# Attention ahead of two expert layers: constant products on TensorE in three of its waits

## The chip, the cores and the metric

One NeuronCore of a Trainium2 chip runs one program from start to end. The metric is the device time of that program in microseconds (us); lower is better. Every time below is from one core, and the rows of the trace are from one profiled execution.

## The reference, cut to what matters

The program computes three things in a row: a gated linear attention (written as a recurrence over 768 steps), and two layers of 8 experts each. Only the first one is touched.

```python
B, H, S, D = q.shape                       # 4, 8, 768, 40
for t in range(S):
    m_new = np.maximum(f_gate[:, :, t] + m, i_gate[:, :, t])
    f_stab = np.exp(f_gate[:, :, t] + m - m_new)
    i_stab = np.exp(i_gate[:, :, t] - m_new)
    m = m_new
    C = f_stab[:, :, None, None] * C + i_stab[:, :, None, None] * np.einsum('bhd,bhe->bhde', vt, kt)
    n = f_stab[:, :, None] * n + i_stab[:, :, None] * kt
    h_tilde = np.einsum('bhde,bhe->bhd', C, qt)
    denom = np.maximum(np.abs(np.einsum('bhd,bhd->bh', n, qt)[:, :, None]), 1.0)
    y[:, :, t] = 1.0 / (1.0 + np.exp(-o_gate[:, :, t])) * h_tilde / denom
...
x = y.transpose(0, 2, 1, 3).reshape(B * S, H * D)      # 3072 tokens x 320
x = moe(x)      # logits = x @ w_gate; tokens to 8 experts of equal size, in order of the logits
return moe2(x)  # logits; each token to its best expert, times its softmax weight
```

## The kernel before, in words

**Stages.** The program is a row of blocks, one after the other, with a barrier between them: a small block that makes the constants (an identity `ident` and a tile of ones `ones_b`, 128x128, bf16), the attention, the first expert layer, the second one. This case is about the attention and about the border to the first expert layer.

**The attention, cut into units.** The 768 steps are worked in 6 chunks of 128 tokens (NC = 6). In each chunk there are 8 units (UPC = 8), one for every four of the 32 batch-head pairs, which makes 48 units. For a unit TensorE does, by its functions' names: `decay_rows` (4 products into `p_G`), `scores` (4 wide products of queries and keys into `p_S`), `outputs` (8 products of scores and values, 4 with the state `C`, 8 for the new state, into `p_O`); after every even unit `x_transposes` (3 transposes of the finished rows `xs` into `p_L`) and after every odd one `logits` (6 small products: the logits of the first expert layer). A matrix product in f32 takes more than one instruction's worth of passes; the trace shows it as a longer one or as two.

**The order.** `step(c, k)` issues, on TensorE: `decay_rows(k + 2)`, `scores(k + 1)`, `outputs(k)`, then the transposes or the logits. `steps` runs two lead-in steps, a loop over the first five chunks, and the last chunk written out. TensorE works strictly in the order in which its instructions are issued. VectorE turns `p_G` into log weights (line 368), ScalarE takes their exponentials (300, 303), GpSimd weights the values and decays the state, VectorE multiplies the scores with the weights (377), and after `outputs` reads the result out (391 to 405), and GpSimd scales it and gates it into `xs` (268, 273). SP loads each next chunk's tiles and stores the finished rows.

**The start.** Ahead of the units the gates are worked into `col`, `G` and `G_parts` by VectorE and GpSimd. TensorE waits for `G` and `col`, transposes both in 12 small transposes (lines 435, 436), and then waits for the rest: the constants, the bf16 parts of `G` (`parts_done`), the copy `colT` (`colT_done`), the exponentials `eG` (`eG_done`, ScalarE, line 328) and the gate weights. Only then do `decay_rows(0)` and the rest follow.

**The end.** After the last unit's `outputs` and `logits` TensorE waits until VectorE and GpSimd have finished the last rows (`y_done`), transposes them (line 495), waits until ScalarE has copied the transposes out (`xT_done`, lines 309 and 310), and multiplies the last logits (line 502). VectorE copies these (line 412), the block ends, and the first expert layer starts with VectorE's `best` (884) and TensorE's pivots (1242), then the counting products (1248).

**Constant products that are there already.** The first expert layer has a function `busy(n)` of its own (line 1239) that multiplies the tile of ones by itself, 512 columns wide, into a bank that nobody reads; it is used inside its search rounds, ahead of its experts and at its end. The second layer has six such products at its start (line 1736).

Of the kernel before, what the change touches and what calls it, by code (L numbers as in the profile page):

```python
# [14 lines left out]
P = 128  # L15
# [5 lines left out]
HU = 4  # L21
# [25 lines left out]
def unit(c, k):  # L47

    return c + k // UPC, k % UPC, c * UPC + k


def wait_done(eng, sem, n):

    eng.wait_ge(sem, n + 1 + LEAD)


def steps(eng, step):

    step(0, -2, False)
    step(0, -1, False)  # L60
    with eng.Fori(0, NC - 1) as c:
        for k in range(UPC):
            step(c, k, False)
    for k in range(UPC):
        step(NC - 1, k, True)
# [42 lines left out]
def attention(nc, a, sh):  # L108

    with ExitStack() as ctx:  # L110
# [27 lines left out]
        p_G, p_S, p_O, p_L = bank[1:3], bank[3:5], bank[5:7], bank[7]  # L138
# [64 lines left out]
        def _(pool):  # L203
# [52 lines left out]
            def decayed_state(c, k):  # L256
                _, k, u = unit(c, k)
                wait_done(pool, eGl_done, u)
                wait_done(pool, C_done, u - QB)
                nc.gpsimd.tensor_tensor(Cd[:, k % QB, :, :], C[:, k, :, :].rearrange("p r (j e) -> p (r j) e", e=V1),  # L260
                                        eGl[:, k % QB, :].unsqueeze(2).to_broadcast([P, HU, V1]), ALU.mult).then_inc(Cd_done, 1)
# [30 lines left out]
        def _(act):  # L292
# [3 lines left out]
            def weights(c, k):  # L296
                _, k, u = unit(c, k)
                wait_done(act, C_done, u - QB)
                wait_done(act, D_done, u)
                nc.scalar.activation(eGl[:, k % QB, :], p_G[k % 2][:, :].rearrange("p (h t) -> p h t", t=P)[:, :, P - 1],  # L300
                                     ACT.Exp).then_inc(eGl_done, 1)
                w = W[:, k % QB, :, :].rearrange("p h t -> p (h t)")
                nc.scalar.activation(w, w, ACT.Exp).then_inc(W_done, 1)
# [29 lines left out]
        def _(dve):  # L333
# [29 lines left out]
            def log_weights(c, k):  # L363
                _, k, u = unit(c, k)
                w = W[:, k % QB, :, :].rearrange("p h t -> p (h t)")
                wait_done(dve, mask_done, u)
                wait_done(dve, G_psum, u)
                nc.vector.tensor_tensor(w, p_G[k % 2][:, :], w, ALU.add).then_inc(D_done, 1)  # L368
# [59 lines left out]
        @block.tensor  # L428
        def _(pe):
            for x in pe_sems:  # L430
                pe.sem_inc(x, LEAD - (x is xT_psum or x is L_psum))
            pe.wait_ge(G_done, 1)
            pe.wait_ge(col_done, 1)
            for c in range(NC):
                nc.tensor.transpose(p_L[:, c * BH:(c + 1) * BH], col[0:BH, c * P:(c + 1) * P], ident[0:BH, 0:BH])
                mm = nc.tensor.transpose(p_L[:, (NC + c) * BH:(NC + c + 1) * BH], G[0:BH, c * P:(c + 1) * P], ident[0:BH, 0:BH])
            mm.then_inc(gates_T, 1)
            pe.wait_ge(consts, 4)
            pe.wait_ge(zeroed, 2)
            pe.wait_ge(parts_done, 3)  # L440
            pe.wait_ge(dg, 3)
            pe.wait_ge(colT_done, 1)
            pe.wait_ge(eG_done, 1)
            pe.wait_ge(in_wg, 16)

            def decay_rows(c, k):

                c, k, u = unit(c, k)
                wait_done(pe, D_done, u - 2)
                wait_done(pe, eGl_done, u - 2)  # L450
                pe.sem_inc(pe_carry, 1)
                for h in range(HU):
                    bh = k * HU + h
                    mm = nc.tensor.matmul(p_G[k % 2][:, h * P:(h + 1) * P], pick_row[:, bh:bh + 1].to_broadcast([3 * BH, P]),
                                          G_parts[:, bass.ts(c, P)], start=True, stop=True)
                mm.then_inc(G_psum, 1)

            def scores(c, k):
                c, k, u = unit(c, k)
                b, par = k // 2, k % 2  # L460
                pe.wait_ge(in_qk[b], c * (16 * QLOADS) + 16 * QLOADS)
                pe.sem_inc(pe_carry, 1)
                wait_done(pe, P_done, u - 2)
                for r in range(PR):
                    pair = k % 2 * PR + r
                    mm = nc.tensor.matmul(p_S[par][:, 2 * r * P:(2 * r + 2) * P], kT[:, b, pair, :],  # L466
                                          qD[:, b, pair, :, :].rearrange("p j t -> p (j t)"), start=True, stop=True)
                mm.then_inc(S_psum, 1)

            def outputs(c, k):  # L470
                u = c * UPC + k
                b, h0, par = k // 2, k % 2 * HU, k % 2
                op = p_O[par]
                wait_done(pe, P_done, u)
                pe.wait_ge(in_v[b], c * 16 + 16)
                wait_done(pe, num_done, u - 2)
                wait_done(pe, C_done, u - 2)
                wait_done(pe, wv_done, u)
                for h in range(HU):
                    nc.tensor.matmul(op[:, h * V1:(h + 1) * V1], Pm[:, par, h, :], v[:, b, h0 + h, :], start=True, stop=True)  # L480
                for r in range(PR):
                    mm = nc.tensor.matmul(op[:, (HU + 2 * r) * V1:(HU + 2 * r + 2) * V1], qT[:, b, k % 2 * PR + r, :], C[:, k, r, :],
                                          start=True, stop=True)
                for h in range(HU):
                    mm = nc.tensor.matmul(op[halves[h % 2], (2 * HU + h // 2) * V1:(2 * HU + h // 2 + 1) * V1],
                                          k_[:, b, (h0 + h) * D:(h0 + h + 1) * D], wv[:, k % QB, h, :], start=True, stop=True)
                mm.then_inc(O_psum, 1)

            def x_transposes(c, k):

                i, b = c * B + k // 2 - 1, (k // 2 - 1) % B
                wait_done(pe, y_done, c * UPC + k - 1)
                wait_done(pe, L_done, i - 1)
                for j, (k0, kn) in enumerate(KT):
                    mm = nc.tensor.transpose(p_L[0:kn, j * P:(j + 1) * P], xs[:, b, k0:k0 + kn], ident[:, :])
                mm.then_inc(xT_psum, 1)

            def logits(c, k):
                i = c * B + k // 2 - 1
                pe.wait_ge(xT_done, 2 * i + 2 + 2 + LEAD - 1)  # L500
                for j, (k0, kn) in enumerate(KT):
                    mm = nc.tensor.matmul(p_L[:, 3 * P:3 * P + NE], xT[0:kn, j, :], wg[0:kn, 0, j, :],
                                          start=j == 0, stop=j == len(KT) - 1)
                mm.then_inc(L_psum, 1)

            def step(c, k, last):
                if not (last and k + 2 >= UPC):
                    decay_rows(c, k + 2)
                if not (last and k + 1 >= UPC) and k + 1 >= 0:
                    scores(c, k + 1)  # L510
                if k >= 0:
                    outputs(c, k)
                    if k % 2 == 0:
                        x_transposes(c, k)
                    else:
                        logits(c, k - 1)

            steps(pe, step)
            x_transposes(NC - 1, UPC)
            logits(NC - 1, UPC)  # L520


# [1389 lines left out]
```

## Time and profile before

| | us |
|---|---|
| three runs | 804.33, 804.60, 815.23 |
| median of the three | 804.6 |
| the profiled execution, its own time | 811.87 |
| its span in the trace | 810.2 |
| TensorE busy, share of the span | 707.8 (87%) |
| VectorE busy | 549.8 (68%) |
| attention, in the span | to about 208.4 |

The span is what the trace covers; 1.7 us of the execution's own time lie outside it. The profiled execution took 7.3 us more than the median of the runs. A busy TensorE says that an instruction was in flight, not that the array worked at its full speed: the same instruction can take twice as long at the lower of its two clock levels (1.2 and 2.4 GHz).

### The profile page before, as it was taken

The page shows a single profiled execution, that of the slowest core. Times are in us where ns is not written, and L with a number is a line of the kernel's source. Part 1 is how long each engine was busy: PE and PEld are TensorE (multiplying, and loading weights), DVE is VectorE, ACT ScalarE, POOL GpSimd, SP SyncE. Part 2 cuts the span into 40 slices and gives each one's busy share as a digit, 9 for nine tenths or more (in the row PEclk, how much of TensorE's full clock was granted, in tenths as well). Part 3 has the DMA queues.
Part 4 walks back from the last instruction along what each step waited for, and adds up shares of the span by engine and source line. Part 5 has one row for each costly group of instructions (what it writes and reads, how often), then busy time and mean ns, then how long its engine had stood idle before and what let it go on. Part 6 is the DMA issues. An engine that isn't in the chain of part 4 may idle for free. (4 is left out here: it accounts for less than half of the span.)

```text
span 810.2 us, 16421 instructions
## 1 busy us (share of the span) xinstructions
PE 707.8 (87%) x4855; PEld 627.9 (78%) x4855; DVE 549.8 (68%) x1666; ACT 294.2 (36%) x743; POOL 341.0 (42%) x484
## 2 busy tenths in 40 slices
PE   0799999999435799888899999987999999999996
PEld 0699999999324695776777887873989899899996
DVE  5569899998677777777888756464536366455652
ACT  4322222222013442241635446451524255344440
POOL 7568887787003322140615326342324134240441
PEclk9999999999557999999999999999999999999998
DMA  8956667761642423231343352344653335451610
GB/s 274 176 155 187 190 184 188 194 187 38 206 124 65 158 80 95 79 119 62 79 136 120 103 173 88 134 145 159 221 157 117 119 108 165 148 164 57 201 35 19
DMA packets 99639, 109.56 MB, mean 135 GB/s; under 512 B 39053, under 2 KB 83726, under 8 KB 99568
## 3 DMA queue, kind: packets, MB, share of 16 engines
q1 hardware_dynamic: 88384, 84.27, 36.2%
q0 software_dynamic: 4080, 12.61, 4.8%
q10 hardware_dynamic: 7104, 11.80, 4.4%
q8 instruction: 36, 0.59, 0.3%
q14 instruction: 35, 0.29, 0.1%
HBM read 89.45 MB, written 20.02 MB: 135 GB/s over the span
## 5 line engine op out<-in xcount | busy, mean ns | idle before, releaser
L566 POOL TENSOR_TENSOR parts_w2l<-all_w,parts_w2h 128x320 fp32r<-128x320 f32 x128 | 111.8, 898 | 275.6 <-ACT parts_w2h L553 275.2
L640 DVE SCALAR_TENSOR_TENSOR l_hl<-bank,l_hh 128x384 fp32r<-128x384 f32 (+1 forms) x138 | 78.0, 566 | 93.4 <-ACT l_hh L636 92.0
L636 ACT ACTIVATE l_hh<-bank 128x384 fp32r<-128x384 f32 (+1 forms) x138 | 69.0, 500 | 132.6 <-PE bank L607 127.9
L603 PE MATMUL bank<-l_xh,parts_w1h 128*128 128x384 f32 x256 | 89.5, 350 | 11.2 <-DVE l_hl L640 9.8
L604 PE MATMUL bank<-l_xl,parts_w1h 128*128 128x384 f32 x256 | 86.3, 337 | 0.0
L605 PE MATMUL bank<-l_xh,parts_w1l 128*128 128x384 f32 x256 | 86.3, 337 | 0.0
L560 DVE TENSOR_TENSOR parts_w1l<-all_w,parts_w1h 128x384 fp32r<-128x384 f32 x128 | 77.6, 638 | 1.1 <-ACT parts_w1h L546 0.7
L627 PE MATMUL bank<-parts_w2h,l_hh 128*128 128x320 f32 x232 | 75.1, 324 | 0.7 <-DVE l_hl L640 0.5
L628 PE MATMUL bank<-parts_w2l,l_hh 128*128 128x320 f32 x232 | 72.3, 312 | 0.0
L629 PE MATMUL bank<-parts_w2h,l_hl 128*128 128x320 f32 x232 | 72.3, 312 | 0.0
L1434 PE MATMUL bank<-parts_w2h,l_hh 128*128 128x320 f32 x192 | 67.5, 351 | 3.5 <-issue 1.9
L603 PEld LDWEIGHTS bank<-l_xh,parts_w1h 128*128 128x128 f32 x256 | 48.1, 188 | 17.2 <-issue 14.1
L1435 PE MATMUL bank<-parts_w2l,l_hh 128*128 128x320 f32 x192 | 60.8, 317 | 0.0
L1436 PE MATMUL bank<-parts_w2h,l_hl 128*128 128x320 f32 x192 | 60.7, 316 | 0.0
L546 ACT ACTIVATE parts_w1h<-all_w 128x384 fp32r<-128x384 f32 x128 | 59.0, 516 | 4.3 <-DMA all_w<-in_moe_w 4.3
L466 PE MATMUL bank<-att_qD,att_kT 128*128 128x256 f32 x192 | 56.4, 420 | 0.0
L588 ACT ACTIVATE l_xh<-bank 128x384 fp32r<-128x384 f32 x48 | 23.5, 491 | 89.2 <-PE bank L582 88.3
L480 PEld LDWEIGHTS bank<-att_v,att_Pm 128*128 128x128 f32 x384 | 53.0, 200 | 2.9
L553 ACT ACTIVATE parts_w2h<-all_w 128x320 fp32r<-128x320 f32 x128 | 55.0, 464 | 0.0
L242 POOL TENSOR_TENSOR att_W<-att_mask,att_colT 128x512 f32<-128x512 f32 x48 | 49.9, 1040 | 1.3 <-issue 1.3
L480 PE MATMUL bank<-att_v,att_Pm 128*128 128x41 f32 x384 | 49.5, 280 | 0.0
L300 ACT ACTIVATE att_eGl<-bank 128x4 f32<-128x4 f32 x48 | 8.4, 175 | 110.7 <-DVE att_W L368 110.7
(269 smaller groups left out, 1728.9 us busy)
## 6 DMA issues: line engine op xcount, KB each, us to landing
all_w<-in_moe_w SPq DMA_DIRECT2D x16, 1024.0 KB, 5.4
all_w<-in_moe_w SPq DMA_DIRECT2D x10, 1280.0 KB
all_w<-in_moe_w SPq DMA_DIRECT2D x32, 256.0 KB, 6.4
all_w<-in_moe_w ACTq DMA_DIRECT2D x6, 1280.0 KB
att_kT<-in_kT SPq DMA_DIRECT2D x24, 256.0 KB, 2.8
att_qD<-in_qT SPq DMA_DIRECT2D x48, 128.0 KB, 3.1
att_qT<-in_qT SPq DMA_DIRECT2D x24, 256.0 KB, 3.2
rows<-parts_pad SPq DMA_DIRECT2D x8, 483.0 KB, 7.1
```

The costliest lines, as they stand in the source:

```text
L480: nc.tensor.matmul(op[:, h * V1:(h + 1) * V1], Pm[:, par, h, :], v[:, b, h0 + h, :], start=True, stop=True)
L560: ops.tensor_tensor(sh.w1l[:, r, :, f], sh.w1[:, :, f], sh.w1h[:, r, :, f].bitcast(FP), ALU.subtract).then_inc(sh.w1_low, 1)
L566: ops.tensor_tensor(sh.w2l[:, r, p, :], sh.w2[:, p, :], sh.w2h[:, r, p, :].bitcast(FP), ALU.subtract).then_inc(sh.w2_low, 1)
L603: T.matmul(dst, sh.w1h[:, r, k, f], xh[:, k, :], start=k == 0, stop=False)
L604: T.matmul(dst, sh.w1h[:, r, k, f], xl[:, k, :], start=False, stop=False)
L605: T.matmul(dst, sh.w1l[:, r, k, f], xh[:, k, :], start=False, stop=False)
L627: T.matmul(dst, hh[:, f, cols], sh.w2h[:, r, f, :], start=f == 0, stop=False)
L628: T.matmul(dst, hh[:, f, cols], sh.w2l[:, r, f, :], start=False, stop=False)
L629: mm = T.matmul(dst, hl[:, f, cols], sh.w2h[:, r, f, :], start=False, stop=f == FT - 1)
L636: return nc.scalar.activation(hh, src, ACT.Relu)
L640: return nc.vector.scalar_tensor_tensor(hl, src, 0.0, hh.bitcast(FP), ALU.max, ALU.subtract)
L1434: T.matmul(dst, hh[:, f, j * P:(j + 1) * P], sh.w2h[:, r, f, :], start=f == 0, stop=False)
```

## The change

TensorE gets a local function `busy(n, bank_)` in the attention, which multiplies the tile of ones by itself, 512 columns wide, into a bank, with no semaphore and no reader. It is called three times: 11 products into `p_O[1]` behind the 12 transposes of the gates and ahead of the waits at the start; 8 into `p_S[0]` between the last `logits` of the last step and the last `x_transposes`; 3 into `p_S[0]` between these and the last `logits`. Nothing else is added, removed or moved.

```diff
+            def busy(n, bank_):
+                for _ in range(n):
+                    nc.tensor.matmul(bank_[:, :], sh.ones_b[:, :], sh.ones_b[:, :].unsqueeze(1).to_broadcast([P, HU, P]),
+                                     start=True, stop=True)
+
             pe.wait_ge(G_done, 1)
             pe.wait_ge(col_done, 1)
             for c in range(NC):
                 nc.tensor.transpose(p_L[:, c * BH:(c + 1) * BH], col[0:BH, c * P:(c + 1) * P], ident[0:BH, 0:BH])
                 mm = nc.tensor.transpose(p_L[:, (NC + c) * BH:(NC + c + 1) * BH], G[0:BH, c * P:(c + 1) * P], ident[0:BH, 0:BH])
             mm.then_inc(gates_T, 1)
+            busy(11, p_O[1])
             pe.wait_ge(consts, 4)
             pe.wait_ge(zeroed, 2)
             pe.wait_ge(parts_done, 3)
@@
             steps(pe, step)
+            busy(8, p_S[0])
             x_transposes(NC - 1, UPC)
+            busy(3, p_S[0])
             logits(NC - 1, UPC)
```

## Rows read from the trace of the kernel before

A row of a timeline gives the start, the busy time of the group in us, the engine, the line, what it writes and reads, how many, and in brackets the idle time ahead of it with what ended it.

**Rows 1.** The page's 40 slices of the span: the granted clock, in tenths

```profile
PEclk9999999999557999999999999999999999999998
```

**Rows 2.** The page's chain that ended last, by engine

```profile
PE 26%; DMA 2%; DVE 1%; issue 1%; ACT 0%; SPq 0%; POOL 0%; DVEq 0%; POOLq 0%; ACTq 0%
```

**Rows 3.** Timeline, all engines, 0 to 42 us: start, us, engine, line, tile, count

```profile
19.87 0.29 PE L436 MATMUL bank<-all_ident,att_G 32*128 32x32 f32 x1
...
24.92 1.01 PE L454 MATMUL bank<-att_G_parts,att_pick_row 96*128 96x128 bf16 x8 [4.77 <-ACT att_eG L328]
...
25.73 2.02 PE L466 MATMUL bank<-att_qD,att_kT 128*128 128x256 f32 x4
...
27.86 0.69 DVE L377 TENSOR_TENSOR att_Pm<-bank,att_W 128x512 f32<-128x512 f32 x1 [0.93 <-PE bank L466]
...
29.78 1.77 PE L480 MATMUL bank<-att_v,att_Pm 128*128 128x41 f32 x8
...
30.42 0.56 SPq L176 DMA_DIRECT2D att_v<-in_v  x1
```

**Rows 4.** Timeline of TensorE, 38 to 50 us

```profile
46.71 1.75 PE L466 MATMUL bank<-att_qD,att_kT 128*128 128x256 f32 x4
48.29 0.98 PE L480 MATMUL bank<-att_v,att_Pm 128*128 128x41 f32 x8
```

**Rows 5.** Timeline of TensorE, 48 to 60 us

```profile
51.06 1.08 PE L466 MATMUL bank<-att_qD,att_kT 128*128 128x256 f32 x4
51.98 0.98 PE L480 MATMUL bank<-att_v,att_Pm 128*128 128x41 f32 x8
...
53.66 0.55 PE L495 MATMUL bank<-all_ident,att_xs 128*128 128x128 f32 x3
...
55.19 0.98 PE L480 MATMUL bank<-att_v,att_Pm 128*128 128x41 f32 x8
...
58.88 0.98 PE L480 MATMUL bank<-att_v,att_Pm 128*128 128x41 f32 x8
```

**Rows 6.** DMA issues in 15 to 50 us, with us to landing

```profile
att_v<-in_v SPq DMA_DIRECT2D x4, 160.0 KB, 6.3
```

**Rows 7.** Timeline of TensorE, 245 to 256 us

```profile
249.03 2.18 PE L582 MATMUL bank<-all_ident,parts_raw 128*128 128x128 f32 x9 [1.86 <-DMA parts_raw<-rows,l_row_i]
251.00 2.81 PE L1239 MATMUL bank<-all_ones_b 128*128 128x512 bf16 x8
```

**Rows 8.** Windows: busy (count) of each engine, PEclk, DMA share, GB/s

```profile
205.00:210.00 5.00, 2.86 (x11) 2.29 (x11) 1.17 (x11) 0.54 (x2) 0.47 (x4) 0.51 0.13 39
210.00:250.00 40.00, 16.12 (x100) 10.51 (x100) 29.08 (x121) 4.58 (x11) 3.09 (x3) 0.50 0.62 187
252.00:253.00 1.00, 1.00 (x5) 0.31 (x3) 0.99 (x3) 0.00 (x0) 0.00 (x0) 0.57 0.00 0
```

**Rows 9.** Line L1239's wide constant products, at either clock

```profile
L1239 PE MATMUL bank<-all_ones_b x4: 589/634/634, 554.5 to 555.8; 128*128 128x512 bf16 x4
...
L1239 PE MATMUL bank<-all_ones_b x25: 379/379/380, 556.7 to 561.8; 128*128 128x512 bf16 x25
```

**Rows 10.** Timeline, all engines, 201 to 216 us

```profile
201.99 0.93 PE L502 MATMUL bank<-all_wg,att_xT 128*128 128x8 f32 x6
...
205.09 0.90 PE L495 MATMUL bank<-all_ident,att_xs 128*128 128x128 f32 x3 [2.17 <-POOL att_xs L273]
...
206.03 0.39 ACT L309 ACTIVATE att_xT<-bank 128x256 f32<-128x256 f32 x1 [4.97 <-PE bank L495]
...
206.62 1.55 PE L502 MATMUL bank<-all_wg,att_xT 128*128 128x8 f32 x6 [0.63 <-ACT att_xT L310]
208.20 0.17 DVE L412 COPY tok_L<-bank 128x8 f32<-128x8 f32 x1 [4.34 <-PE bank L502]
...
209.59 0.80 PE L1242 MATMUL bank<-all_ident,l_pivot 128*128 128x128 f32 x2 [1.42 <-DVEq L893]
...
212.33 3.58 PE L1248 MATMUL bank<-l_above,l_choice 128*8 128x128 bf16 x24 [1.95 <-DVE l_above L915]
```

## The prediction

> **What bounds the kernel now.** I read the page first, where the granted clock, in 40 slices, is far below full only in slices 11 to 13 [rows 1]. The chain that ended last is no help here: it covers about a third of the span [rows 2] and none of it is in the attention, so the stretches have to be read from the timelines. The reader is to compare durations of one and the same group. At 25.73 the four score products of a unit take 2.02 us [rows 3]; at 51.06 the same four take 1.08 [rows 5]. That is the lower of the two clock levels against the upper one, although the clock row shows full speed there. Where the two disagree I trust the durations, since every group of the first units is slow by the same share. At 46.71 the group takes 1.75 [rows 4], part slow and part fast: the clock came up near 47.9. From 24.92, when the last gate wait ended (4.77 us of idle, released by ScalarE's eG [rows 3]), to 47.9 TensorE was thus busy without a gap, at half its clock: 23 us. In this stretch TensorE is the bound. The second slow stretch begins at the end of the attention: 205 to 210 shows 0.51, so the clock fell at about 205.1 [rows 8], after the 2.17 us of idle ahead of the last transposes [rows 10], and in 210 to 250 it stands at 0.50 [rows 8]; 252 to 253 has 0.57, so it came back near 252.9 [rows 8].
>
> **What the fillers cost.** The same product stands in the trace already, on line 1239. At the slow level it takes 634 ns from start to end, and four of them start from 554.5 to 555.8, about 0.42 us apart (with one small product between the first two); at the fast level it is 379 ns, and 25 start from 556.7 to 561.8, 5.1/24 = 0.21 us apart [rows 9].
> Start: the 12 transposes of the gates are issued by 19.98 (the last one starts at 19.87 [rows 3], they come 0.11 apart). Eleven fillers at the slow level are 11 x 0.42 = 4.6 us, issued until 24.6; the last one drains by 24.8. The next real product starts at 24.92 [rows 3]. So they fit with 0.1 us, and take less if the clock rises under them. Cost taken: 0; bounds 0 to 0.3. Nothing else waits for TensorE there: the transposes' semaphore is raised ahead of the fillers, and the bank p_O[1] is first needed by outputs(1).
> End, eight fillers: the last logits end at 201.99 + 0.93 = 202.92, the transposes start at 205.09 [rows 10]. At the fast level eight need 8 x 0.21 = 1.7 us, done by 204.8 with the drain. Cost 0. At the slow level they would need 3.4 us and make the transposes 1.2 to 1.4 us late.
> End, three fillers: transposes end at 205.99, logits start at 206.62, 0.63 us later [rows 10]. At the fast level three are 0.63 us, issued under the drain of the transposes; cost 0 to 0.15. At the slow level they are 1.26 us, 0.6 to 0.8 late.
>
> **What the start gives.** If the clock is up when the units begin, they run as they do later. From outputs(0) at 29.78 [rows 3] to outputs(3) at 48.29 [rows 4] three units took 18.51 us. Later an even unit takes 55.19 - 51.98 = 3.21 and an odd one 58.88 - 55.19 = 3.69 [rows 5]. From unit 0 to unit 3 there are two even ones and one odd one: 3.21 + 3.69 + 3.21 = 10.11. Gain 18.51 - 10.11 = 8.4 us. Behind outputs(3) both are fast already, and what is late next is what bounds the later units now, TensorE still.
> Ahead of it, from 24.92 to 29.78, TensorE's part is two groups of decay rows and two of scores. Here other engines come in: VectorE's first Pm (line 377) starts at 27.86 and takes 0.69 [rows 3], so it is there at 28.55, and its chain (decay rows, log weights, exponentials, weighted values) shortens only by what the first decay rows give, about 0.25. Outputs(0) could then start near 28.4 to 28.9. Gain between 0.3 and 1.4, taken 1.0, nearer to the upper end because scores(1) on TensorE and not Pm was what came last.
> The inputs could stand in the way: the fourth batch's values are issued at 30.42 [rows 3], a load lands 6.3 us later here [rows 6], so at about 37; in the faster order units 6 and 7, which need that batch, come near 28.9 + 6 x 3.45 = 50 (their scores one unit sooner). Cost 0.
> Sum of the start: 8.4 + 1.0 = 9.4. Bounds: the clock may rise late, some microseconds into the units, each costing 0.45 us per us; with one slow stretch as long as those that I see around wide products (249.03, where the work ahead of the experts starts, to 252.9: 3.9 us [rows 7, 8]) counted from 24.9, it is 3.9 x 0.45 = 1.8 less. So 7.5 to 10.
> Does it rise at all? At 249.03 nine transposes and then eight fillers of line 1239 start at the slow level, and the clock is up at 252.9 [rows 7, 8]. At 554.5 fillers run slow, and from 556.7 on fast [rows 9]. The start has 12 transposes and 4.6 us of the same fillers, so about 6 us without a gap. What speaks against it is that the units kept TensorE busy for 23 us before it came up: being busy isn't enough. But the fillers stream 512 columns into every start, the units mostly 41 to 256 behind a weight load each.
> The Trainium skill, "TensorE: Matmul & The Clock Gate", Part 1 (what is actually happening), says that the default is the throttled clock and that sustained activity releases it, and elsewhere in Part 1 that the ramp is under 1% of a typical span. By the first, the units would have released it by themselves soon and the start would give next to nothing (rival A); this trace disagrees, with 23 us. By the second the ramp would be worth at most 8 us, and the time 811.9 - 8 - 1.2 = 802.7; the rows give 9.4.
>
> **What the end gives.** With the clock kept up over the wait, the transposes take 0.55, as those of the loop at 53.66 [rows 5], in place of 0.90 [rows 10], ScalarE's copy (206.03 [rows 10]) starts 0.35 earlier, and the logits take 0.93 in place of 1.55, the same six products at 201.99 and 206.62 [rows 10]: 0.62. VectorE's last copy (208.20) moves by 0.97, and all of this is on the path, since the next layer can't start sooner. Behind it, TensorE idles again, about 1.4 us to 209.59 [rows 10]. The pivots (0.80) could still run fast, a gain of 0 to 0.3; the counting at 212.33 comes after another 1.95 us of idle and is fed by VectorE, whose comparisons last as long. Taken 0.2. Sum of the end 1.2, bounds 0.5 to 1.6.
>
> **The sum.** 9.4 + 1.2 = 10.6 us. Against the profiled execution, 811.9 - 10.6 = 801.3. That execution is 7.3 us above the median of the runs, and what it lost there isn't shown. Two readings. If the median runs came up earlier than 47.9, they have part of the gain already, and the changed kernel, which is up from the start in any run, lands at 801.3. If the 7.3 us lie elsewhere (in the execution under the profiler, or in the short slow stretches of the expert layers), it is 804.6 - 10.6 = 794.0. The slow start is the only stretch that is long enough to hold 7.3 us, and the unit groups there differ from run to run in nothing but the clock, so I give the first reading three quarters: 794.0 + 0.75 x 7.3 = 799.5. The two readings are the two ends of the forecast.
>
> **The rivals.**
> A. The units come up by themselves. In the runs that make the median, the clock rises a few microseconds after 24.92, and what the fillers save is part of one such short stretch (1.8 us at most, 1.0 taken) beside the 1.2 of the end. Time 804.6 - 1.0 - 1.2 = 802.4. For it: the fast runs are 7.3 us under the profiled one, which would be 16 us of slow clock at 0.45. Against it: it asks that the marginal activity of the units suffices in two runs of three. What the Trainium skill says on sustained activity (the page and part named above) describes this case.
> B. The fillers do what they say and the clock doesn't hold. The first units have gaps: TensorE waits for Pm once it is fast, some 0.5 to 0.9 us before outputs(0), and a fall there would begin the slow stretch anew, with up to 23 us of it. Then the start gives 1 to 3 us, 2 taken: 804.6 - 2.0 - 1.2 = 801.4, or 808.7 if the slow start is in the profiled time alone.
> C, the slower side. The fillers do not lift the clock, or not while they run, and the end is at the slow level: the eleven end 0 to 0.3 late, the eight 1.2 to 1.4 late, the three 0.6 to 0.8 late. That is 804.6 + 0.2 + 1.3 + 0.7 = 806.8. It decides where eleven wide products are too few for the chip. The fall at 205 despite full work until 202.9 speaks for some caution; the rises at 252 and 556 under the same product speak against it.
> D. Everything behind is shifted, and the clock's falls in the expert layers, which come at waits of 1 to 7 us, fall differently. A slow stretch of 3.9 us costs 1.8; two more or fewer give 3.6 us of either sign, so 799.5 becomes 803.1 or 795.9.
> E. The clock stays up over the border and into the search rounds of the first layer, where TensorE is busy 16.12 of 40 us at the slow level [rows 8]; at most half of that comes off, 8 us. TensorE mostly waits for VectorE there (29.08 of 40 busy). It would be 790 or so.
>
> **How the numbers follow.** Chances: forecast with both readings 0.62, A 0.12, B 0.08, C 0.10, D at its far ends 0.05, E 0.03. The predicted time is 799.5. The range goes from 794.0 less the 1.3 of the late terms' bounds to the far side of A, B and half of C: 792.7 to 805.0, which leaves out E, most of C and the ends of D, some 0.15 to 0.2. 2% of 804.6 is 16 us, about what a measurement of this kernel can tell from no change; the whole of the gain is 1.3% and only E together with the second reading (804.6 - 10.6 - 8 = 786) gets beyond it: faster 0.04. Slower by 16 us has no mechanism that I can name: 0.01. Within 2%: 0.95.
>
> **What the profile would show.** Eleven products of 512 columns between 20.0 and 24.9, the first ones 0.42 us apart and, if the clock rises under them, the last ones 0.21; decay rows at 24.9 or a little later; the four score products of the first units at 1.08 and not 2.02; outputs(0) near 28.5, outputs(3) near 39; the attention's end near 198 in place of 208.4. At the end the last transposes 0.55 and the last logits 0.93 long, and a fall of the clock not before the pivots. I am wrong if the first units still take 2.02 for their scores, if outputs(3) comes after 42, or if the runs stand where they stood while the profiled time falls by 10.

## The result, and the profile after

| | before | changed |
|---|---|---|
| median of 20 runs, us | 803.87 | 800.37 |
| lowest and highest, us | 800.30, 815.23 | 798.47, 802.13 |
| the profiled execution, us | 811.87 | 799.81 |

The ratio changed to before is 0.9952, with a 95% interval of 0.9931 to 0.9973: 0.5% faster, clear of zero and far below 2%. Runs more than 1.5% above the fastest of their kernel are left out of this ratio (two of the 20 before, none of the changed kernel). The spread says more than the median: 14.9 us before against 3.7 us of the changed kernel.

The page of the changed kernel, for comparison with [rows 1] and the table of before:

```profile
span 798.1 us, 16465 instructions
...
PE 704.7 (88%) x4877; PEld 622.8 (78%) x4877; DVE 551.5 (69%) x1666; ACT 293.5 (37%) x743; POOL 341.7 (43%) x484
...
PEclk9999999999557999999999999999999999999998
```

Slices 11 to 13 are still the only ones far below full clock. As before, the page doesn't show the slow first units at all; the timeline of TensorE does. These are the start of the attention and its first units in the changed kernel (line 435 is the filler, 461 the decay rows, 473 the scores, 487 the outputs):

```profile
19.65 3.98 PE L435 MATMUL bank<-all_ones_b 128*128 128x512 bf16 x11
24.48 0.61 PE L461 MATMUL bank<-att_G_parts,att_pick_row 96*128 96x128 bf16 x8 [0.85 <-ACT att_eG L328]
24.93 1.08 PE L473 MATMUL bank<-att_qD,att_kT 128*128 128x256 f32 x4
...
28.25 1.06 PE L487 MATMUL bank<-att_v,att_Pm 128*128 128x41 f32 x8 [0.54 <-DVE att_Pm L377]
...
38.42 0.98 PE L487 MATMUL bank<-att_v,att_Pm 128*128 128x41 f32 x8
```

The eleven fillers take 3.98 us from the first start to the last end; at the slow level they would need 10 x 0.42 + 0.63 = 4.8, so the clock came up under them. The decay rows start at 24.48, 0.85 us behind the fillers' end. The first scores take 1.08 in place of 2.02 [rows 3], outputs(3) stands at 38.42 in place of 48.29 [rows 4]. Counted from the first decay rows, that is 13.94 us in place of 48.29 - 24.92 = 23.37.

The end of the attention and the border, all engines:

```profile
193.09 1.90 PE L435 MATMUL bank<-all_ones_b 128*128 128x512 bf16 x8
...
195.32 0.55 PE L502 MATMUL bank<-all_ident,att_xs 128*128 128x128 f32 x3 [0.33 <-POOL att_xs L273]
...
195.70 0.81 PE L435 MATMUL bank<-all_ones_b 128*128 128x512 bf16 x3
195.74 0.94 SPq L184 DMA_DIRECT2D rows<-att_xs  x1
195.90 0.38 ACT L309 ACTIVATE att_xT<-bank 128x256 f32<-128x256 f32 x1 [4.61 <-PE bank L502]
...
196.49 0.93 PE L509 MATMUL bank<-all_wg,att_xT 128*128 128x8 f32 x6
197.46 0.17 DVE L412 COPY tok_L<-bank 128x8 f32<-128x8 f32 x1 [3.36 <-PE bank L509]
...
198.43 0.35 DVE L893 TENSOR_REDUCE l_best<-tok_L 128x24 f32<-128x192 f32 x1 [0.81 <-PEq L110]
...
199.25 0.49 PE L1251 MATMUL bank<-all_ident,l_pivot 128*128 128x128 f32 x2 [1.83 <-DVEq L902]
...
201.99 3.57 PE L1257 MATMUL bank<-l_above,l_choice 128*8 128x128 bf16 x24 [2.25 <-DVE l_above L924]
```

The eight fillers end at 193.09 + 1.90 = 194.99, 0.33 us ahead of the transposes. These take 0.55 in place of 0.90, the last logits 0.93 in place of 1.55, and from the transposes' start to VectorE's copy of the logits it is 197.46 - 195.32 = 2.14 us in place of 208.20 - 205.09 = 3.11 [rows 10]: 0.97 us, as worked out. But between the copy's end and the next layer's first reduction (198.43) there are now 0.8 us, where it was 0.4; the run store_act below shows what fills them. From the transposes to the pivots the gain is 4.50 - 3.93 = 0.57. The pivots are fast (0.49 for 0.80), the counting at 201.99 is not (3.57, as before). The clock in three windows, with the columns of [rows 8]:

```profile
199.00:200.00 1.00, 0.49 (x2) 0.30 (x2) 0.77 (x5) 0.00 (x0) 0.00 (x0) 1.00 0.29 102
200.00:201.00 1.00, 0.00 (x0) 0.00 (x0) 0.82 (x3) 0.00 (x0) 0.00 (x0) 0.54 1.03 350
244.00:245.00 1.00, 0.96 (x5) 0.79 (x5) 0.97 (x3) 0.00 (x0) 0.00 (x0) 0.77 0.00 0
```

It fell in the microsecond from 200, behind the pivots and not ahead of the last transposes, and came back late in the one from 244, 5.9 us after the row tiles began (238.57); before it was 3.9.

### The profile page after: what moved, and what is told of

Same layout as the page of the kernel before. It is cut to its first block and busy times, and to the rows that moved or that the text cites. A ratio compares the mean times of both kernels' runs of the same rounds, so it can differ in the third digit from the quotient of the medians.

```text
span 798.1 us, 16465 instructions
## 1 busy us (share of the span) xinstructions
PE 704.7 (88%) x4877; PEld 622.8 (78%) x4877; DVE 551.5 (69%) x1666; ACT 293.5 (37%) x743; POOL 341.7 (43%) x484
## 5 line engine op out<-in xcount | busy, mean ns | idle before, releaser
L597 ACT ACTIVATE l_xh<-bank 128x384 fp32r<-128x384 f32 x48 | 23.4, 490 | 88.8 <-PE bank L591 87.9
L487 PEld LDWEIGHTS bank<-att_v,att_Pm 128*128 128x128 f32 x384 | 50.3, 191 | 3.3 <-issue 0.9
L473 PE MATMUL bank<-att_qD,att_kT 128*128 128x256 f32 x192 | 52.0, 393 | 0.0
L613 PEld LDWEIGHTS bank<-l_xl,parts_w1h 128*128 128x128 f32 x256 | 48.8, 190 | 0.1
L614 PEld LDWEIGHTS bank<-l_xh,parts_w1l 128*128 128x128 f32 x256 | 48.5, 189 | 0.0
```

Source lines behind the costliest of these rows:

```text
L613: T.matmul(dst, sh.w1h[:, r, k, f], xl[:, k, :], start=False, stop=False)
L614: T.matmul(dst, sh.w1l[:, r, k, f], xh[:, k, :], start=False, stop=False)
```

## The experiments

Twelve runs. Before the numbers, one table which holds their main reading: for every profiled execution, the time from the first decay rows to outputs(3), from the last transposes to the pivots, and the time of that execution.

| kernel | products added at the start | to outputs(3), us | transposes to pivots, us | profiled time, us | runs above 809 |
|---|---|---|---|---|---|
| before (first profile) | none | 23.37 | 4.50 | 811.87 | 19 of 107 |
| before_again | none | 14.27 | 4.49 | 803.42 | |
| before_third | none | 23.38 | 4.36 | 812.59 | |
| end_only | none | 23.47 | 3.52 | 810.17 | 1 of 13 |
| start_narrow | 42 of 32 columns | 15.37 | 4.14 | 803.71 | 2 of 12 |
| start_reload | 42 of 32 columns | 15.46 | 4.13 | 804.06 | 2 of 12 |
| start_f32 | 20 in f32, 8 columns | 23.50 | 4.27 | 813.54 | 3 of 12 |
| start_four | 4 of 512 | 23.46 | 4.46 | 812.96 | 2 of 12 |
| changed kernel | 11 of 512 | 13.94 | 3.93 | 799.81 | 0 of 20 |
| after_again | 11 of 512 | 13.94 | 4.32 | 799.46 | 0 of 12 |
| start_only | 11 of 512 | 13.94 | 4.15 | 800.43 | 0 of 12 |
| start_double | 22 of 512 | 13.94 | 4.50 | 800.95 | 0 of 12 |
| border_busy | 11 of 512 | 13.94 | 3.93 | 803.31 | 0 of 12 |
| store_act | 11 of 512 | 13.94 | 3.83 | 801.62 | 0 of 12 |

"Before" has 107 timed runs: 20 with the result, and 35, 29 and 23 with the experiments; the 17 more beside store_act are told there. Between 807.84 and 810.64 no run of them lies: it is 88 in one group with a median of 803.15 (the early group below), and 19 in another with a median of 812.31 (the late group). All fourteen profiled executions fit this: the five that reach outputs(3) 23.37 us or more behind the decay rows (no kernel with eleven fillers is among them) took 810.17 to 813.54, the other nine 799.46 to 804.06.

**The kernel before, again, twice.**

> The kernel before, word for word, once more, for its trace. In the runs so far it falls into two groups, 800 to 806 and 810.6 to 815. Theory (when the clock comes up under the first units differs from run to run, early near 30 us or late near 48 us in the span, and this is what parts the groups): outputs(3) at about 40 to 41 in a run of about 803, and at 48 in one of about 812. Rival (the first units are always slow until 48, and the groups come from elsewhere): 48 in either.

> The kernel before, word for word, for one more trace. Theory: outputs(3) is about 14 to 16 us behind the first decay rows if the run is of the group near 803 (81 of 100), and 23 if it is near 812; no other value.

The two runs took 803.42 and 812.59 us. The timeline of TensorE in the first (line 454 decay rows, 466 scores, 480 outputs):

```profile
24.99 1.01 PE L454 MATMUL bank<-att_G_parts,att_pick_row 96*128 96x128 bf16 x8 [4.77 <-ACT att_eG L328]
25.80 2.02 PE L466 MATMUL bank<-att_qD,att_kT 128*128 128x256 f32 x4
...
28.03 1.30 PE L466 MATMUL bank<-att_qD,att_kT 128*128 128x256 f32 x4
29.17 0.98 PE L480 MATMUL bank<-att_v,att_Pm 128*128 128x41 f32 x8
...
39.26 0.98 PE L480 MATMUL bank<-att_v,att_Pm 128*128 128x41 f32 x8
```

The first scores are slow (2.02), the second group takes 1.30, so the clock came up by itself near 28.5, and outputs(3) is at 39.26. In the second, outputs(3) is at 48.30, as in the profile that the prediction was made from. So the same program has two starts, 9.1 us apart, and its two groups of runs are 9.2 us apart (812.31 - 803.15). That is shown. The program is the same word for word, so nothing in it decides between the two; by their times, 88 of 107 runs get the early one. My number for outputs(3) in the early group, 40 to 41, was a little late: it was 39.3.

**The start alone.**

```diff
-            busy(8, p_S[0])
...
-            busy(3, p_S[0])
```

> The changed kernel without the eight and the three products at the end; the eleven at the start stay. Theory (the start carries the gain, the end about 1 us or less): units at the fast clock from the first one, outputs(3) within 10.5 us of outputs(0), a time 0.5 to 1.2 us above the changed kernel's 800.4, about 801.2. Rival (the end carries most of the measured 3.5 us): within 1 us of the kernel before.

Median 800.57 of twelve runs, 799.04 to 802.08, ratio 0.9963 (0.9942 to 0.9985). The first units are fast: outputs(3) comes 39.06 - 28.89 = 10.17 us behind outputs(0). The narrow spread comes from the start: over all kernels with eleven or more fillers there, 0 of 80 runs are above 809, over those without (the kernel before apart), 10 of 61. The expected loss of 0.5 to 1.2 us against the changed kernel is too small to be decided: the medians are 800.57 against 800.37 and 800.92, while the kernel before beside them differs by 1.1 us (804.08 with start_only, 803.87 and 802.99 with the other two). The theory stands on the start; on the end this run is silent.

**The end alone.**

```diff
-            busy(11, p_O[1])
```

> The changed kernel without the eleven products at the start; the eight and the three at the end stay. Theory: the units' clock comes up by itself at a time that differs from run to run, so the runs are spread as wide as those of the kernel before (800 to 815 there) and their median is 0.5 to 1.2 us below it. Last transposes 0.55, last logits 0.93, the next layer's pivots at the fast level. Rival (the end carries most): near 800.5, and a narrow spread.

Median 801.39 of thirteen, 800.12 to 803.41 and one of 810.17; ratio 0.997 (0.995 to 0.9989). The late run is back, so the fillers at the end do nothing against it, and this is the run whose trace was taken. Its border, all engines:

```profile
205.05 0.55 PE L501 MATMUL bank<-all_ident,att_xs 128*128 128x128 f32 x3 [0.33 <-POOL att_xs L273]
...
205.47 0.43 SPq L184 DMA_DIRECT2D rows<-att_xs  x1
...
206.23 0.93 PE L508 MATMUL bank<-all_wg,att_xT 128*128 128x8 f32 x6
...
207.76 0.35 DVE L892 TENSOR_REDUCE l_best<-tok_L 128x24 f32<-128x192 f32 x1 [0.40 <-PEq L110]
...
208.57 0.67 PE L1250 MATMUL bank<-all_ident,l_pivot 128*128 128x128 f32 x2 [1.42 <-DVEq L901]
```

From the transposes (205.05) to the pivots (208.57) it is 3.52 us in place of 4.50: here the whole 0.98 arrived. The first reduction starts 207.76 - (207.19 + 0.17) = 0.40 behind the copy, as in the kernel before. Its median is 1.8 us below the early group's 803.15, more than the trace's 1.0; the rest isn't explained. The rival (the end carries most) expected a narrow spread near 800.5; the median alone wouldn't have told the two apart, the one late run and the trace do.

**Twenty-two at the start.**

```diff
-            busy(11, p_O[1])
+            busy(22, p_O[1])
```

> Start only, with 22 products of 512 columns. The clock should rise under them as in the changed kernel, at about the eighth; the other eleven or more take 0.21 us each and end near 25.8 in place of 23.6, where the wait ends at 24.5. Theory (the eleven are hidden by the wait with under 1 us to spare): 1 to 1.5 us slower than start_only. Rival (the fillers cost nothing whatever their number, since the wait for other engines is longer): same as start_only within 0.3.

Median 802.74, 800.95 to 808.13: 2.2 us slower than start_only, ratio to before 0.9999 (0.9975 to 1.0022). TensorE's timeline:

```profile
20.45 6.27 PE L435 MATMUL bank<-all_ones_b 128*128 128x512 bf16 x22
26.55 0.61 PE L461 MATMUL bank<-att_G_parts,att_pick_row 96*128 96x128 bf16 x8
...
30.32 1.06 PE L487 MATMUL bank<-att_v,att_Pm 128*128 128x41 f32 x8 [0.54 <-DVE att_Pm L377]
```

The fillers end at 26.72 and the decay rows follow at once at 26.55, where start_only has them at 25.12: 1.4 us late, as expected, and the units behind are shifted by just that. So eleven fit and twenty-two don't. The rival (they cost nothing whatever their number) is out. The other 0.7 us of the difference (2.17 - 1.43) isn't in the start.

**Narrow products.**

```diff
-            busy(11, p_O[1])
+            for _ in range(42):
+                nc.tensor.matmul(p_O[1][:, 0:32], sh.ones_b[:, :], sh.ones_b[:, 0:32], start=True, stop=True)
```

> Start only, with 42 constant products of 32 columns in place of eleven of 512: TensorE is as busy for about 4.5 us, and streams a quarter of the columns. Theory (columns streamed, not being busy, bring the clock up early): the first units run slow, scores at 2.02 and not 1.08, and the runs are spread like those of the kernel before, 800 to 815. Rival (a busy TensorE is enough): the first units are fast and the time is that of start_only, about 801, narrow.

This missed its aim. TensorE's timeline:

```profile
20.08 1.30 PE L445 MATMUL bank<-all_ones_b 128*128 128x32 bf16 x42
...
25.73 2.02 PE L474 MATMUL bank<-att_qD,att_kT 128*128 128x256 f32 x4
...
27.96 2.02 PE L474 MATMUL bank<-att_qD,att_kT 128*128 128x256 f32 x4
...
40.29 0.98 PE L488 MATMUL bank<-att_v,att_Pm 128*128 128x41 f32 x8
```

The 42 products were over in 1.30 us, not 4.5, about 0.027 us apart, and 3.54 us of idle followed; so neither the columns nor the busy time were those of eleven wide ones. Two of twelve runs stand above 809, as often as before; median 801.61, ratio 0.9975 (0.9939 to 1.0011). It says that so short a stretch isn't enough, and nothing on which of the two counts.

**Narrow products with a weight load each.** The weights alternate between `sh.ones_b` and `sh.before_b`; the rest is as above.

> Start only, with 42 constant products of 32 columns whose weights alternate between two tiles, so that each has a weight load: TensorE is occupied for about 4.5 us (0.11 us each) and streams a quarter of the columns that eleven wide ones do. (The 42 products of the run before this one, with one tile of weights, took 1.3 us in all, and so didn't test this.) Theory (columns streamed count): no early rise from them; two groups of runs as before, median 802 to 804.5. Rival (being busy counts): every run in one narrow group at 800.5.

It failed in the same way: a bf16 weight load between two such products doesn't spread them, they start about 0.027 us apart (20.22, 20.24, 20.27 and so on). Two of twelve runs are above 809, the median is 802.5, the ratio 0.9991 (0.9952 to 1.003).

**Busy, with few columns.**

```diff
-            busy(11, p_O[1])
+            for _ in range(20):
+                nc.tensor.matmul(p_O[1][:, 0:8], ident[:, :], ident[:, 0:8], start=True, stop=True)
```

> Start only, with 20 constant products of the identity in f32, 8 columns each, the shape of the logits products. In the trace of the kernel before six of these take 1.55 us at the slow clock, so 20 occupy TensorE for about 5 us with 160 columns in place of 5632. This is the control that the two runs with 32 columns, which were over in 1.3 us, didn't give. Theory (columns count, not being busy): the first units stay slow at least until unit 0, one or more of twelve runs near 811, median 802 to 804. Rival (busy is enough): scores at 1.08 from the first unit, no run above 806, median 800.5.

TensorE's timeline:

```profile
20.08 8.70 PE L445 MATMUL bank<-all_ident 128*128 128x8 f32 x40
28.63 1.01 PE L462 MATMUL bank<-att_G_parts,att_pick_row 96*128 96x128 bf16 x8
29.44 2.02 PE L474 MATMUL bank<-att_qD,att_kT 128*128 128x256 f32 x4
...
52.13 0.98 PE L488 MATMUL bank<-att_v,att_Pm 128*128 128x41 f32 x8
```

Each f32 product is two instructions, so it was 40 of them and 8.70 us of a TensorE without a gap, well above the 5 us that I wanted, and the units start 3.7 us late. After all of that the clock is still low: the first scores take 2.02, those of later units too, and outputs(3) comes 23.50 us behind the decay rows, as in the late runs of the kernel before. Three of twelve runs are above 809 (812.98 to 813.54); median 805.16, ratio 1.0031 (1.0 to 1.0063). The theory's median of 802 to 804 didn't count the delay. This is the control that works: in this trace 8.7 us without a gap, with 320 columns in all, did not lift the clock; the eleven wide ones, 3.9 to 4.9 us with 5632 columns, did in each of the five traces that have them, and so did the twenty-two. So a busy TensorE alone didn't do it. The two kinds of product differ in their columns and in their type (f32 against bf16), and no run tells which of these matters.

**Four wide ones.**

```diff
-            busy(11, p_O[1])
+            busy(4, p_O[1])
```

> Start only, with four wide products of 512 columns in place of eleven, about 1.7 us of them. Theory (wide work has to go on until the units begin): not enough, clock up during unit 0 at the earliest, median 801.5 to 803, a late run possible. Rival (a short burst is enough): same as start_only, 800.6, no late run.

```profile
20.29 1.89 PE L435 MATMUL bank<-all_ones_b 128*128 128x512 bf16 x4
25.12 1.01 PE L461 MATMUL bank<-att_G_parts,att_pick_row 96*128 96x128 bf16 x8 [2.95 <-ACT att_eG L328]
25.93 2.02 PE L473 MATMUL bank<-att_qD,att_kT 128*128 128x256 f32 x4
...
48.58 0.98 PE L487 MATMUL bank<-att_v,att_Pm 128*128 128x41 f32 x8
```

1.89 us of wide products and then 2.95 us of idle: the first scores are slow and outputs(3) is at 48.58. Two of twelve are above 809, median 803.58, ratio 1.0007 (0.9976 to 1.0038): the kernel before, in effect, and a little above the 801.5 to 803 that the theory gave. The run changes two things at once, the number of products and the idle time behind them, so it doesn't say which of the two was wanting. How many between four and eleven would do wasn't tried.

**The changed kernel again, and with fillers in the next layer's first waits.** The edit of the second, in the lead-in of the first expert layer (its own `busy` writes a bank that is unused there):

```diff
                 pivots()
+                busy(7)
                 pe.wait_ge(choices_ready, k + 1)
...
                         count(i)
+                        busy(1)
                     codes()
+                    busy(8)
...
+                    busy(2)
...
+                    else:
+                        busy(1)
                 codes()
+                busy(9)
                 any_inside()
+                busy(2)
...
                 if k < AHEAD - 1:
+                    busy(8)
                     totals(k)
+                    busy(8)
...
+            busy(4)
             for j in range(CT):
                 row_tile(0, j)
-            busy(8)
+            busy(2)
```

> The changed kernel once more, on the same chip as the others of this call. Expected 800.4, all runs between 798 and 803, no group at 810.

> The changed kernel with constant products also in the waits of the first layer's lead-in (behind the pivots, between the counts, behind the codes, around the totals, and four ahead of the first row tiles in place of eight behind them, of which two stay). Theory: the clock stays up over the border; the three pivots take 0.5 in place of 0.8, the tail of each counting group 0.2 less, list_rows 0.6 less, the row tiles 1.0 less: 2.5 to 3.5 us faster than the changed kernel. Rival (the stage is VectorE's and the fillers delay what follows them): same or up to 1 us slower.

The changed kernel took 800.92 (799.46 to 802.89), ratio 0.995 (0.9916 to 0.9984). The other took 803.98 (801.18 to 808.6), 3 us slower, ratio to before 1.0003. TensorE's timeline there:

```profile
200.04 2.93 PE L1248 MATMUL bank<-all_ones_b 128*128 128x512 bf16 x7
202.90 0.60 PE L1257 MATMUL bank<-l_above,l_choice 128*8 128x128 bf16 x4
...
221.71 3.60 PE L1248 MATMUL bank<-all_ones_b 128*128 128x512 bf16 x8 [1.67 <-issue]
225.10 0.21 PE L1300 MATMUL bank<-l_counts,all_ones_b 128*128 128x1 bf16 x1
...
243.00 1.97 PE L591 MATMUL bank<-all_ident,parts_raw 128*128 128x128 f32 x9
```

The clock is mostly up in this stage now (0.86 of full speed on average from 200 to 243, where the changed kernel has 0.50 from 199.7 to 238.5), and still the stage is longer: pivots to row tiles 43.29 us in place of 39.32. The fillers are in the way. Seven behind the pivots took 2.93 us, some at the slow level, and pushed the first counts from 2.74 us behind the pivots to 3.19 (202.90 - 199.71); eight ahead of the totals started at 221.71 and took 3.60, all slow, and the totals (225.10) came 5.76 us behind the any_inside product (219.34 in that trace) in place of 3.63. The rival was right in kind, though it gave at most 1 us and it was 3: the stage is VectorE's, and a filler that meets the slow level outlasts the wait for which it was counted at the fast one.

**The last store from another queue.** In both traces of the changed kernel SP's issue of the second half of the last row store is long (0.94 us at 195.74; and the second trace below), where it is 0.43 in the kernel before and in end_only, and the border is late in these two. Border_busy has both as well (0.94 us; 0.81 us from the copy to the reduction). Start_double has the long issue (0.93) and not the late border (0.40), but there the logits aren't early. The lines of after_again:

```profile
196.22 1.33 SPq L184 DMA_DIRECT2D rows<-att_xs  x1
...
199.30 0.35 DVE L893 TENSOR_REDUCE l_best<-tok_L 128x24 f32<-128x192 f32 x1 [1.20 <-PEq L110]
```

In this trace VectorE's copy ended at 198.11, so the reduction is 1.2 us behind it. The edit:

```diff
-                sp.dma_start(rows[:, DM:], xs[:, b, 2 * P:]).then_inc(X_in[b], 16)
+                if not last:
+                    sp.dma_start(rows[:, DM:], xs[:, b, 2 * P:]).then_inc(X_in[b], 16)
...
             steps(act, step)
+            wait_done(act, y_done, NC * UPC - 1)
+            act.dma_start(sh.xs1[(NC - 1) * P + (B - 1) * S:N, :][:, DM:], xs[:, B - 1, 2 * P:]).then_inc(X_in[B - 1], 16)
             copy_xT(NC - 1, UPC)
```

> The changed kernel with the second half of the very last row store issued by ScalarE, ahead of its copy of the transposes, in place of SP. In two traces of the changed kernel SP's issue of it took 0.94 and 1.33 us in place of 0.43, and the border to the next layer came 0.4 and 0.8 us late. Theory (SP's late issue holds the border once the logits are early): from the last transposes to the pivots 3.5 us in place of 3.9 and 4.3, median 0.3 to 0.8 us below the changed kernel's 800.4 to 800.9. Rival (the border is held by something else, or ScalarE's issue delays its copies by as much): 3.9 to 4.3 us, same median or worse.

Median 801.46 (799.09 to 803.93), ratio 0.9979 (0.9963 to 0.9994); the kernel before, in the 17 runs beside it, 803.07 and none above 804.93, so that its own 0 of 12 above 809 says little. Its lines:

```profile
195.72 0.38 ACTq L332 DMA_DIRECT2D rows<-att_xs  x1
...
195.77 0.33 SPq L183 DMA_DIRECT2D rows<-att_xs  x1
...
198.75 0.35 DVE L896 TENSOR_REDUCE l_best<-tok_L 128x24 f32<-128x192 f32 x1 [0.71 <-PEq L110]
...
199.57 0.80 PE L1254 MATMUL bank<-all_ident,l_pivot 128*128 128x128 f32 x2 [1.73 <-DVEq L905]
```

Both issues are short, ScalarE's copies aren't delayed, and the border still takes 0.70 us behind the copy (which ended at 198.05), so 3.83 from transposes to pivots. The theory expected 3.5 and a lower median and got neither: the border is late without SP's long issue too.

What holds the border is in the same traces: when the stores have landed. At the end of the block SP waits for both halves (line 200), and the next layer starts behind that. The last issues in the changed kernel and in store_act, with us from issue to landing:

```profile
rows<-att_xs SPq DMA_DIRECT2D x1, 32.0 KB, 2.1
...
rows<-att_xs SPq DMA_DIRECT2D x1, 160.0 KB, 2.4
```

| trace | last store landed, us | reduction started, us | between |
|---|---|---|---|
| changed kernel | 195.74 + 2.1 = 197.84 | 198.43 | 0.59 |
| after_again | 196.22 + 2.5 = 198.72 | 199.30 | 0.58 |
| border_busy | 196.20 + 2.1 = 198.30 | 198.90 | 0.60 |
| store_act | 195.77 + 2.4 = 198.17 | 198.75 | 0.58 |
| end_only | 205.47 + 1.6 = 207.07 | 207.76 | 0.69 |

In the first four the reduction follows the landing by the same 0.6 us, whoever issued the store. In end_only the landing takes 1.6 us, as in the kernel before, and the reduction follows the copy by 0.40 instead; the landing was then 0.1 us from being the last. So once the logits are early, the store's landing is next in line, and by these rows any that takes over about 1.7 us shows in the time. Why it takes 2.1 to 2.5 us in these four traces and 1.6 in others isn't shown.

## Why the prediction held, point by point

**The time.** 799.5 was forecast, 800.37 measured, inside 792.7 to 805.0; within 2%, as expected. That it is so close is in part luck. The profiled execution was costed at 801.3 and took 799.81: 12.1 us less than before. Up to the pivots it had gained 209.59 - 199.25 = 10.3 (of which 0.44 because the first decay rows stood at 24.48 and not at 24.92, which no filler does); the rest, 1.7, lies behind, where next to nothing was forecast. And the pull towards 794.0, from a reading that was false, brought the number to the same distance from the median on its other side (0.9 below in place of 0.9 above).

**The cost of the fillers.** Eleven at the start: 0, with 0.85 us to spare in the trace where the clock came up under them. In after_again they took 4.86, which is the slow level from end to end (4.8), and the decay rows followed at 24.92, where they would have started anyway. Start_double confirms it from the other side. The eight and the three at the end: 0 in the timeline, as counted at the fast level.

**The gain of the start, 9.4 us against the profiled execution.** 23.37 - 13.94 = 9.43 in the traces, 8.34 of it from outputs(0) to outputs(3) (forecast 8.4) and 1.09 ahead of outputs(0) (forecast 1.0). The term was right to a tenth, and so was the mechanism: the early fast clock, with TensorE the bound of the first units, and Pm last for one short gap (TensorE waits 0.54 us for it at 28.25; I had 0.5 to 0.9).

**How it stands to the median.** Here the prediction had two readings and gave three quarters to the first, "the median runs came up earlier than 47.9". That reading is now shown: the profiled execution was of the late kind, like 19 of the 107 timed runs. The second reading, which stood for 794.0, is out. For the typical run the start is worth 14.27 - 13.94 = 0.3 us against before_again, and 1.4 to 1.5 against a rise as late as in start_narrow and start_reload. The quarter that I gave to the second reading pulled the forecast 1.8 us below 801.3.

**Rival A** said the same of the median runs in other words (the units come up by themselves, 1.0 us of gain at the start) and came to 802.4. Its mechanism is what happens in four runs of five. The trace counted against it only because it showed the fifth. The forecast and this rival weren't two cases; they were one, seen from two executions, and the chances that I gave to them apart (0.62 and 0.12) have no meaning beside each other.

**The gain of the end, 1.2 us.** 0.97 up to VectorE's copy, to the hundredth; 0.98 arrives in end_only, but 0.57 in the changed kernel and 0.18 in after_again, since the border is late there. The term was over-sized on two counts. The prediction said that all of the 0.97 is on the path, since the next layer can't start sooner, and so took for granted that nothing else at the barrier was close behind the logits; the landing of the last row store was, 0.1 us behind at best. And it costed the end from one trace, in which the clock had fallen ahead of the transposes; without fillers there the stretch took 4.13 to 4.50 in eight other traces, and in start_only, start_narrow and start_reload the transposes were fast (0.55) without any.

**What the sum leaves.** Against the early group's 803.15 the trace accounts for 0.3 to 1.5 at the start and 0.2 to 1.0 at the end, 0.5 to 2.5 us; the medians differ by 2.2 to 2.8 (800.92 and 800.37). Up to 2 us may lie in the expert layers: from the first up product to the second layer's first transposes it is 308.1 to 308.6 us in the changed kernel, after_again, start_only and start_double, but 310.0 in store_act and 310.4 in border_busy; without the eleven it is 309.9 to 311.9 in seven traces and 308.4 in the eighth. Nothing in the change touches this stretch, and the kernel before, unchanged, has 308.4 in one of its traces and 310.3 in the next, so the change can't be credited with it from these traces. No run isolates it, and it stays open: of the typical run's gain, up to 2 us have no shown cause.

**Rivals B, C, D, E.** B (the clock doesn't hold): no trace with eleven wide fillers lost it in the first units. C (not lifted): in none. D: slow stretches in the expert layers do differ from trace to trace. E (up over the border) came true for the pivots only, and border_busy shows that forcing it costs 3 us.

## What to carry to other kernels

When one program's runs fall into two groups, take the trace of one run of each before costing a change: a profile may be of the rare group, and a gain that is right against it (9.4 us here) can be several times what the typical run has to give (0.3 to 1.5). To lift TensorE's clock ahead of work that is full of small products, eleven wide products that ended at most 1.0 us ahead of the work did it here, and a busy engine alone didn't; count them at the slow level wherever the clock can be low when they start. Put them only into waits that are longer than that. And before counting an end that comes earlier as a gain, look at what else the next stage waits for: here a store's landing was 0.1 us behind.

## What the runs showed of the hardware that was not expected

- The granted clock of the page and of the windows reads 1.00 through the whole slow start, as in this window of the kernel before, in which the scores take 2.02 (us, busy and count of PE, PEld, DVE, ACT and POOL, then the clock): ahead of the first fall that it shows, it doesn't tell the level. The durations of one repeated group are the measure.

```profile
29.70:47.90 18.20, 18.20 (x96) 16.29 (x95) 8.59 (x28) 2.88 (x9) 7.50 (x14) 1.00 0.65 151
```

- Left to itself, the clock came up under the first units at one of a few places: in the eight traces without eleven wide products, outputs(3) stood 14.3, 15.4 or 15.5, or (five times) 23.4 to 23.5 us behind the first decay rows, even where the units began 3.7 us later (start_f32). So in these five traces the late rise came at the same piece of work, not at the same time of the span (start_f32 alone has the units at another time).
- 40 f32 instructions with 8 columns kept TensorE busy for 8.70 us and the clock low; bf16 products of 32 columns start about 0.027 us apart, whether they share their weights or not.
